# Narrow expert program first and with the rest of the kernel inside its branch; attention scores as 64x64 tiles from the keys as loaded

## The chip, the cores and the metric

The kernel runs on one core of a Trainium2 chip. A core has five engines with instruction queues of their own: TensorE (PE, matrix products; its weight loads are shown as PEld), VectorE (DVE), ScalarE (ACT), GpSimd (POOL) and SyncE (SP, which here only issues DMAs). They meet by semaphores alone. On-chip data lies in SBUF (128 partitions); matrix products go to PSUM (8 banks of 512 fp32 per partition). The metric is the device time of one execution in microseconds.

## What is computed

Three layers in fp32. First a linear attention with a decayed state (B, H, S, D = 2, 8, 768, 48):

```python
for t in range(S):
    cur = np.einsum('bhd,bhe->bhde', u[None] * kt, vt)
    y[:, :, t] = np.einsum('bhd,bhde->bhe', rt, state + cur)
    state = w[None, :, :, None] * state + np.einsum('bhd,bhe->bhde', kt, vt)
```

Its 1536 tokens of 384 features go to a mixture of 8 experts (384 to 1024 and back, relu), each token to the expert of its largest gate logit, at most 384 tokens an expert, times its gate probability:

```python
h = np.maximum(np.einsum('ecd,edf->ecf', disp, w1), 0.0)
y = np.einsum('ecf,efd->ecd', h, w2)
out[i] = gate_w[i] * y[expert_idx[i], pos[i]]
```

Last comes a dense layer over all tokens, 384 to 2048 and back:

```python
h = x @ w_in
r = np.maximum(h, 0.0)
return ((r * r) @ w_out).astype(np.float32)
```

## The kernel before

**Attention** goes over 12 chunks of 128 tokens (6 for each of 2 batches, in turn; four slots of buffers). For a chunk, POOL multiplies the keys in place by a table of decays (L376, k_decayed) and writes the decayed r to Rd (L377, r_decayed), then khat (L383) and ru (L385). Heads lie in pairs: the one on partitions 0 to 47, the other on 64 to 111. ACT copies the decayed keys to Kb, where each head of a pair has a block of its own with zeros in the other's partitions (two copies a chunk, kb_ready; Kb[0] is cleared once by DVE at L773, Kb[1] by POOL at L370). PE then makes vT x wg (L445, three products), the scores (L451, eight fp32 products, 112 partitions deep and 128 x 128 large, into two banks ps_a), the new state (L459) and the outputs (L467, L469). DVE masks the scores to am (L828, one operation for each bank), makes ru, csum and cv (L832, L833, L835), takes the outputs out of PSUM (x_sb L821, heads_l L839) and adds up the states St (L845). PE's L459 waits for St of the chunk before, L467 for am, DVE's L821 for L469. An fp32 product stands in the trace as two weight loads and two matmuls (passes): "x16" is eight products.

**Routing** follows on DVE and PE: positions, the gather indices gidx, the number of tokens of the fullest expert (peaki, L895, count_ready) and each expert's first column (starti, L898).

**The experts** exist as two programs: wide, for experts of up to 384 tokens, and narrow, for up to 240. Every engine but SP reads peaki into a register and branches (by_peak, L280); these inputs take the narrow program. In `moe` POOL gathers each expert's tokens (L393) and, behind the gathers of expert 1, clears the compact arrays yhi and ylo (L412, L413; 128 x 4608 each). The expert outputs are written there column range by column range, 240 or 384 wide, in the order of experts, so that a later expert overwrites what the one before wrote past its own tokens. PE starts with matmuls that only keep it busy (warm: L543, 18 and 6), and transposes the first gathered rows (L592). ACT copies them to xshi, DVE makes the difference xslo (L993). DVE's part starts with gates() (L902 to L906) and the first weight split (L812: wlo = raw - whi), and then come xslo 0 to 2, splits 1 and 2 and the first hlo (L952). For each of 32 units (a quarter of an expert) PE does a hidden product of 18 matmuls (L504) and an output product of 18 (L517), the hidden product one unit ahead. SP loads the weights of a unit (raw, 768 KB) into a ring of four as soon as DVE has split the ones that lay there (w_lo).

**The dense layer** has 24 units over yhi and ylo (L504, L527). Last, POOL scatters the 12 output tiles (L421) and waits for them. This part and the placing matmuls (L616) stand behind the branch, where both programs meet.

The branch reads:

```python
            with eng.If(biggest > NARROW):
                moe(Experts(CAP))
            with eng.Else():
                moe(Experts(NARROW))
```

Of the kernel before, what the change touches and what calls it, by code (L numbers as in the profile page):

```python
# [20 lines left out]
P = 128  # L21
# [36 lines left out]
SLOTS = 4  # L58
NARROW = 240
# [3 lines left out]
def build(nc, feat_d, vT_d, rk_d, vx_d, w_d, u_d, wg_d, wts_d, xd, out):  # L63
    with ExitStack() as ctx:
# [48 lines left out]
        with ExitStack() as a:  # L113
# [5 lines left out]
            Kb = [sb(f"Kb{u}", [P, G, 2, C], F32, a) for u in range(2)]  # L119
# [29 lines left out]
        bank = [ctx.enter_context(nc.psum_tensor(f"bank{j}", [P, 512], F32)) for j in range(8)]  # L149
        ps_a0, ps_a1, ps_y, ps_kv, ps_x, _, ps_tab, ps_tab2 = bank  # L150
        ps_pos = ps_kv
        ps_a = [ps_a0, ps_a1]
# [29 lines left out]
        kb_cleared = sem("kb_cleared")  # L182
        kb_ready = sem("kb_ready")
# [96 lines left out]
        def by_peak(eng, moe):  # L280
# [61 lines left out]
        def _(pool):  # L342
# [27 lines left out]
            nc.gpsimd.memset(Kb[1][:, :, :, :], 0.0).then_inc(kb_cleared, 1)  # L370
# [44 lines left out]
            by_peak(pool, moe)  # L415

            pool.wait_ge(place_ready, 2)
            pool.wait_ge(out_zeroed, 16 * NT)
            for t in range(NT):
                pool.wait_ge(o_dve if t % 2 else o_act, t // 4 * 2 + t % 4 // 2 + 2)  # L420
                nc.gpsimd.indirect_dma_start(  # L421
                    out=out[:, :], out_offset=bass.IndirectOffsetOnAxis(ap=oidx[:, t:t + 1], axis=0),
                    in_=osb[:, t, :], in_offset=None, bounds_check=N - 1, oob_is_err=False).then_inc(scattered, 16)
            pool.wait_ge(scattered, 16 * NT)
# [3 lines left out]
        def _(pe):  # L428
# [9 lines left out]
            with pe.Fori(0, NC_ // 2) as i:  # L438
                for u in range(SLOTS):
                    n, b = 4 * i + u, u % 2  # L440

                    pe.wait_ge(in_vT[u], 16 * (i + 1))
# [20 lines left out]
                    for g in range(G):  # L463
# [4 lines left out]
                        for o in range(2):  # L468
                            mm = pe.matmul(pair, am[:, g // 2, (2 * (g % 2) + o) * C:(2 * (g % 2) + o + 1) * C],  # L469
# [141 lines left out]

            pe.wait_ge(count_ready, 1)
            by_peak(pe, moe)
            for t in range(NT):
                pe.wait_ge(onehot, NT + t + 1)
                mm = pe.matmul(ps_tab2[:, 0:PARTS * NT], onehb[:, t, :], tokv[:, t, :, :].rearrange("p a t -> p (a t)"),  # L616
                               start=(t == 0), stop=(t == NT - 1))
            mm.then_inc(tab_psum, 1)

            def mlp_chunk(t, last):  # L620
                for v in range(MQ):
                    n = MOE_UNITS + MQ * t + v
                    if not (last and v == MQ - 1):
                        pe.wait_ge(w_lo, n + 2)
                        hidden((v + 1) % RING, ps_h[(v + 1) % 2], *compact(t + (v + 1) // MQ), CHUNK)
                    pe.wait_ge(h_ready, 2 * n + 2)
                    if v == 0:
# [470 lines left out]
```

## Time and profile before

| | us |
|---|---|
| median of 3 runs | 461.97 |
| lowest and highest | 461.69, 467.37 |
| profiled execution | 461.56 |
| span of its instructions | 459.8 |
| PE busy in the span | 424.0 (92%) |
| DVE busy | 295.8 (64%) |
| ACT busy | 212.1 (46%) |
| POOL busy | 103.0 (22%) |

The profiled execution takes 461.56 us in all, of which 459.8 us lie between its first and last instruction. All times in the rows are counted from the start of that span. A timeline row reads: start, duration, engine, line, operation, written tile <- read tiles, shape, xcount; in square brackets, how long the engine had been idle and what ended that ("issue": nothing that the profile shows). A matmul's duration holds its way through the array; the distance of two starts is what each costs.

### The profile page before, as it was taken

The numbers are of one execution on the slowest core, as the hardware profiler recorded it, in microseconds if no ns is written. First come the engines' busy times: TensorE is split into PE (matmuls) and PEld (weight loads), VectorE is DVE, ScalarE is ACT, GpSimd is POOL, SyncE is SP. The second block draws the span as 40 slices with busy tenths as digits, with TensorE's granted clock in tenths as the row PEclk, the third lists the DMA queues.
The fourth block names the chain that finished last, engine by engine and source line by source line (L and its number), as shares of the span: only waits on it lengthen the run. The fifth ranks groups of instructions, "written<-read, shape, count | busy, mean of one in ns | idle before, by whom it ended". The sixth has DMA issues, their size and how long they took to land.

```text
span 459.8 us, 8053 instructions
## 1 busy us (share of the span) xinstructions
PE 424.0 (92%) x2922; PEld 399.4 (87%) x2922; DVE 295.8 (64%) x486; ACT 212.1 (46%) x371; POOL 103.0 (22%) x102
## 2 busy tenths in 40 slices
PE   2999999644999999999999999999999999999993
PEld 2999989623999999999999889889899899898993
DVE  8799988759678766676865755455554554554431
ACT  2554665301465555655653644444543445444321
POOL 6998865057101101100000000000300001100003
PEclk9999999957899999999999999999999999999998
DMA  7999982012996456455546323122432142300001
GB/s 201 273 321 296 344 262 112 35 55 65 309 364 227 160 217 233 173 200 199 202 165 209 113 71 136 68 97 110 137 118 88 68 133 93 117 0 1 1 1 69
DMA packets 20477, 69.48 MB, mean 151 GB/s; under 512 B 2840, under 2 KB 9257, under 8 KB 20448
## 3 DMA queue, kind: packets, MB, share of 16 engines
q1 hardware_dynamic: 18656, 64.40, 42.2%
q0 software_dynamic: 1792, 4.72, 2.7%
q8 instruction: 15, 0.25, 0.2%
q14 instruction: 14, 0.11, 0.1%
HBM read 62.82 MB, written 7.08 MB: 152 GB/s over the span
## 4 chain that ended last, share of the span: by engine, by line
PE 79%; DVE 14%; issue 4%; DVEq 1%; POOL 0%; ACT 0%; DMA 0%; ACTq 0%; POOLq 0%
PE bank L504 34%; PE bank L527 22%; PE bank L517 13%; PE bank L469 3%; DVE ru L832 2%; PE bank L451 2%; DVE r_sum L904 2%; PE bank L467 1%; DVE am L828 1%; PE bank L459 1%; DVE cv L835 1%; DVE St L845 1%; PE bank L494 1%; DVE wlo L812 1%; PE bank L445 1%
## 5 line engine op out<-in xcount | busy, mean ns | idle before, releaser
L812 DVE TENSOR_TENSOR wlo<-raw,whi 128x1536 fp32r<-128x1536 f32 x56 | 98.3, 1757 | 91.8 <-ACT whi L642 87.5
L642 ACT ACTIVATE whi<-raw 128x1536 fp32r<-128x1536 f32 x56 | 83.3, 1489 | 83.2 <-PE bank L527 47.6
L421 POOL DMA_INDIRECT out<-osb,oidx x12 | 13.0, 1080 | 247.8 <-ACT osb L755 245.4
L527 PE MATMUL bank<-whi,hhi 128*128 128x384 f32 x192 | 65.0, 338 | 0.5 <-DVE hlo L962 0.5
L527 PE MATMUL bank<-whi,hlo 128*128 128x384 f32 x192 | 64.9, 338 | 0.0
L527 PE MATMUL bank<-wlo,hhi 128*128 128x384 f32 x192 | 64.8, 338 | 0.0
L504 PE MATMUL bank<-xshi,whi 128*128 128x240 f32 x192 | 53.9, 281 | 6.5 <-DVE xslo L993 6.5
L504 PE MATMUL bank<-yhi,whi 128*128 (+1 forms) x144 | 56.9, 395 | 0.0
L504 PE MATMUL bank<-yhi,wlo 128*128 (+1 forms) x144 | 56.9, 395 | 0.0
L504 PE MATMUL bank<-ylo,whi 128*128 (+1 forms) x144 | 56.8, 395 | 0.0
L504 PE MATMUL bank<-xslo,whi 128*128 128x240 f32 x192 | 53.8, 280 | 0.0
L504 PE MATMUL bank<-xshi,wlo 128*128 128x240 f32 x192 | 53.8, 280 | 0.0
L699 ACT ACTIVATE rl<-bank 128x512 f32<-128x512 f32 x48 | 28.6, 600 | 54.5 <-PE bank L504 51.0
L958 DVE TENSOR_TENSOR sq<-rl 128x512 f32<-128x512 f32 x48 | 32.9, 689 | 30.0 <-ACT rl L699 30.0
L504 PEld LDWEIGHTS bank<-xshi,whi 128*128 128x128 f32 x192 | 37.4, 195 | 6.8 <-DVE wlo L812 6.8
L393 POOL DMA_INDIRECT xg<-attention_out,gidx x16 | 18.3, 1142 | 93.1 <-PE bank L494 69.0
L527 PEld LDWEIGHTS bank<-whi,hhi 128*128 128x128 f32 x192 | 36.0, 188 | 1.9 <-issue 0.9
L504 PEld LDWEIGHTS bank<-xshi,wlo 128*128 128x128 f32 x192 | 37.3, 194 | 0.0
L504 PEld LDWEIGHTS bank<-xslo,whi 128*128 128x128 f32 x192 | 37.3, 194 | 0.0
L527 PEld LDWEIGHTS bank<-wlo,hhi 128*128 128x128 f32 x192 | 36.0, 188 | 0.9
L527 PEld LDWEIGHTS bank<-whi,hlo 128*128 128x128 f32 x192 | 36.0, 188 | 0.0
L517 PE MATMUL bank<-hhi,whi 128*128 128x240 f32 x192 | 33.0, 280 | 0.0
(158 smaller groups left out, 794.6 us busy)
## 6 DMA issues: line engine op xcount, KB each, us to landing
raw<-in_wts SPq DMA_DIRECT2D x56, 768.0 KB, 4.2
feat<-in_feat SPq DMA_DIRECT2D x12, 448.0 KB, 6.4
rk<-in_rk SPq DMA_DIRECT2D x12, 384.0 KB, 5.9
vx<-in_vx SPq DMA_DIRECT2D x12, 224.0 KB, 6.5
vT<-in_vT SPq DMA_DIRECT2D x12, 192.0 KB, 6.0
attention_out<-x_sb SPq DMA_DIRECT2D x12, 192.0 KB, 2.8
out<-rl SPq DMA_DIRECT2D x12, 192.0 KB
xg<-attention_out,gidx POOLq DMA_INDIRECT x16, 4.7
```

The lines of the kernel that those rows point to most:

```text
L393: nc.gpsimd.indirect_dma_start(out=xg[e % 2][:, q, :], out_offset=None, in_=xd[:, :], in_offset=bass.IndirectOffsetOnAxis(ap=gidx[:, e * C ...
L421: nc.gpsimd.indirect_dma_start(out=out[:, :], out_offset=bass.IndirectOffsetOnAxis(ap=oidx[:, t:t + 1], axis=0), in_=osb[:, t, :], in_offs ...
L451: mm = pe.matmul(ps_a[g // 2][:, (2 * (g % 2) + o) * C:(2 * (g % 2) + o + 1) * C], Kb[u % 2][0:ROWS, g, o, :], Rd[u][0:ROWS, g * C:(g + 1) ...
L469: mm = pe.matmul(pair, am[:, g // 2, (2 * (g % 2) + o) * C:(2 * (g % 2) + o + 1) * C], vb[u % 2][:, g, o, :], start=False, stop=(o == 1))
L504: mm = pe.matmul(banks[ft][:, 0:width], w[:, r, cols], x(k), start=(k == 0 and step == 0), stop=(k == KT - 1 and step == 2))
L517: mm = pe.matmul(ps_e[dt][:, 0:width], w[:, r, cols], x[:, par, ft, 0:width], start=(q == 0 and ft == 0 and step == 0), stop=(q == EQ - 1 ...
L527: mm = pe.matmul(ps_o[tt][:, 0:DM], x[:, par, ft, tt * P:(tt + 1) * P], w[:, r, cols], start=(v == 0 and ft == 0 and step == 0), stop=(v = ...
L642: return nc.scalar.activation(dst, src, ACT.Copy)
L699: nc.scalar.activation(rl[:, ft, :], banks[ft][:, :], ACT.Relu).then_inc(h_relu, 1)
L812: v.tensor_tensor(wlo[:, r, :], raw[:, r, :], whi[:, r, :].bitcast(F32), ALU.subtract).then_inc(w_lo, 1)
L832: after(v.tensor_tensor(ru[u][:, :], ru[u][:, :], rk[u][:, 1, :], ALU.mult))
L958: v.tensor_tensor(sq[:, ft, :], rl[:, ft, :], rl[:, ft, :], ALU.mult).then_inc(h_sq, 1)
```

## The change

1. In by_peak the narrow program stands first, directly behind the compare, and the wide one behind it. All that follows the experts (placing, dense layer, scatter) moves into a function `rest(x)` on each engine, called inside both branches, so it exists twice.
2. POOL clears yhi and ylo only in the wide program, and only there does ACT wait for it (y_cleared).
3. Kb, its two clears and its ACT copies are gone. PE takes the scores from the keys as decayed in place (feat): for each pair of heads and each head the product is split in two of 64 key columns. A product uses 48 partitions (from 0 or from 64) and writes 64 PSUM partitions (0 to 63 or 64 to 127); the two heads write to different banks. Scores so take 16 products and four banks. The mask reads two banks in one operation. PE waits for k_decayed and r_decayed ahead of the first product of the chunk.
4. The other attention banks move accordingly (ps_tab to bank 1, ps_y, ps_kv and ps_x to 4, 5 and 6).

```diff
-        ps_a0, ps_a1, ps_y, ps_kv, ps_x, _, ps_tab, ps_tab2 = bank
+        ps_a = [ctx.enter_context(nc.psum_tensor(f"score_banks{j}", [P, 2, 512], F32)) for j in range(2)]
+        bank = [ps_a[j][:, o, :] for j in range(2) for o in range(2)]
+        bank += [ctx.enter_context(nc.psum_tensor(f"bank{j}", [P, 512], F32)) for j in range(4, 8)]
+        _, ps_tab, _, _, ps_y, ps_kv, ps_x, ps_tab2 = bank
...
-            with eng.If(biggest > NARROW):
-                moe(Experts(CAP))
+            with eng.If(biggest < NARROW + 1):
+                rest(Experts(NARROW))
             with eng.Else():
-                moe(Experts(NARROW))
+                rest(Experts(CAP))
...
-            nc.gpsimd.memset(Kb[1][:, :, :, :], 0.0).then_inc(kb_cleared, 1)
...
-                    if e == 1:
+                    if e == 1 and x.tiles > 2:
                         nc.gpsimd.memset(yhi[:, :, 0:N].bitcast(F32), 0.0).then_inc(y_cleared, 1)
                         nc.gpsimd.memset(ylo[:, :, 0:N].bitcast(F32), 0.0).then_inc(y_cleared, 1)
...
+                    pe.wait_ge(k_decayed, n + 1)
+                    pe.wait_ge(r_decayed, n + 1)
                     pe.wait_ge(in_vT[u], 16 * (i + 1))
...
-                    pe.wait_ge(kb_ready, 2 * n + 2)
-                    pe.wait_ge(r_decayed, n + 1)
                     for g in range(G):
-                        for o in range(2):
-                            mm = pe.matmul(ps_a[g // 2][:, (2 * (g % 2) + o) * C:(2 * (g % 2) + o + 1) * C],
-                                           Kb[u % 2][0:ROWS, g, o, :], Rd[u][0:ROWS, g * C:(g + 1) * C], start=True, stop=True)
+                        for half in (slice(0, HALF), slice(HALF, P)):
+                            for o in range(2):
+                                rows = slice(ODD * o, ODD * o + D)
+                                mm = pe.matmul(ps_a[g // 2][half, o, (g % 2) * C:(g % 2 + 1) * C],
+                                               feat[u][rows, 1, g * C + half.start:g * C + half.stop],
+                                               Rd[u][rows, g * C:(g + 1) * C], start=True, stop=True)
...
-                for o in range(2):
-                    rows = slice(ODD * o, ODD * o + D)
-                    copy(Kb[u % 2][rows, :, o, :], chunk_view(feat[u][rows, 1, :])).then_inc(kb_ready, 1)
...
-                    act.wait_ge(y_cleared, 2)
+                    if x.tiles > 2:
+                        act.wait_ge(y_cleared, 2)
...
-            v.memset(Kb[0][:, :, :, :], 0.0).then_inc(kb_cleared, 1)
...
-                    v.tensor_tensor(chunk_view(am[:, o, :]), chunk_view(ps[:, :]),
-                                    before[:, :].unsqueeze(1).to_broadcast([P, G, C]), ALU.mult).then_inc(masked, 1)
+                    v.tensor_tensor(am[:, o, :].rearrange("p (o g s) -> p o g s", o=2, g=2),
+                                    ps[:, :, 0:2 * C].rearrange("p o (g s) -> p o g s", g=2),
+                                    before[:, :].unsqueeze(1).unsqueeze(1).to_broadcast([P, 2, 2, C]), ALU.mult).then_inc(masked, 1)
```

PE's program in a chunk of attention, before (bank stands for any PSUM bank):

```order
L445 MATMUL bank<-wg,vT 128x64 x3
L447 ISA
L451 MATMUL bank<-Rd,Kb 128x128 x8
L456 REGISTER_ALU
L459 MATMUL bank<-vx,khat 112x112 x4
```

and in the changed kernel:

```order
L448 MATMUL bank<-wg,vT 128x64 x3
L454 MATMUL score_banks<-Rd,feat 64x128 x16
L460 REGISTER_ALU
L461 ISA
L463 MATMUL bank<-vx,khat 112x112 x4
```

Eight products of full size became sixteen of half the columns. What PE finds behind the branch on the peak count, before (384 is the width of the wide program; the narrow one comes 658 rows further down):

```order
L282 TENSOR_LOAD peaki
L282 ISA x2
L283 COMPARE_AND_BRANCH
L543 MATMUL bank<-match,ones_b 128x288 x18
L592 MATMUL bank<-ident,xg 128x128 x6
L543 MATMUL bank<-match,ones_b 128x288 x6
L603 MATMUL bank<-ident,xg 128x128 x3
L504 MATMUL bank<-xshi,whi 128x384
```

and in the changed kernel, where the narrow program (240) is there at once:

```order
L281 TENSOR_LOAD peaki
L281 ISA x2
L282 COMPARE_AND_BRANCH
L547 MATMUL bank<-match,ones_b 128x288 x18
L596 MATMUL bank<-ident,xg 128x128 x6
L547 MATMUL bank<-match,ones_b 128x288 x6
L508 MATMUL score_banks<-xshi,whi 128x240
```

The same swap stands on DVE, ACT and POOL. POOL's program behind its branch in the changed kernel; the clears of yhi and ylo stand in the wide part, behind the jump to the end:

```order
L282 COMPARE_AND_BRANCH
L391 DMA xg<-attention_out,gidx 128x384 x14
L420 DMA out<-osb,oidx 1536x384 x12
L282 UNCONDITIONAL_BRANCH
L391 DMA xg<-attention_out,gidx 128x384 x4
L410 MEMSET yhi 128x3x1536
L411 MEMSET ylo 128x3x1536
```

The narrow part now ends in the scatters and a jump over the wide part.

## Rows read from the trace of the kernel before

**Rows 1.** Busy time by stage: stretch, length, busy us (count) by engine, clock, DMA.
```profile
9.80:88.00 78.20, 75.46 (x648) 74.39 (x648) 68.38 (x128) 40.28 (x106) 56.69 (x48) 1.00 0.79 245
96.40:112.45 16.05, 5.50 (x30) 3.73 (x31) 11.07 (x8) 0.94 (x3) 14.80 (x9) 0.71 0.18 52
119.40:253.50 134.10, 133.91 (x1181) 132.50 (x1179) 93.11 (x158) 75.65 (x127) 11.35 (x10) 1.00 0.63 218
258.60:452.40 193.80, 193.78 (x972) 175.72 (x972) 97.08 (x118) 84.25 (x118) 10.49 (x10) 1.00 0.23 78
```

**Rows 2.** Timeline of the handoff from routing to the experts, all engines.
```profile
95.70 0.15 DVE L895 CAST peaki<-peak 128x1 int32<-128x1 f32 x1
...
96.27 0.17 DVE L898 CAST starti<-start 128x8 int32<-128x8 f32 x1
...
100.43 3.80 PEld L543 LDWEIGHTS bank<-match,ones_b 128*128 128x128 bf16 x18 [5.60 <-issue]
...
101.29 0.25 DVE L902 TENSOR_REDUCE r_sum<-ex 128x12 f32<-128x96 f32 x1 [4.84 <-issue]
101.58 8.14 DVE L904 TENSOR_SCALAR r_sum<-r_sum 128x12 f32<-128x12 f32 x1
101.85 3.95 POOL L412 MEMSET yhi<- 128x4608 f32 x1
...
104.38 0.82 PE L592 MATMUL bank<-ident,xg 128*128 128x128 f32 x6
...
105.02 0.94 ACT L642 ACTIVATE xshi<-bank 128x256 fp32r<-128x256 f32 x3 [13.32 <-PE bank L592]
...
110.21 1.76 DVE L812 TENSOR_TENSOR wlo<-raw,whi 128x1536 fp32r<-128x1536 f32 x1
...
111.89 1.08 DVE L993 TENSOR_TENSOR xslo<-bank,xshi 128x256 fp32r<-128x256 f32 x3
...
112.45 0.54 PE L504 MATMUL bank<-xshi,whi 128*128 128x240 f32 x1 [6.52 <-DVE xslo L993]
...
119.39 0.58 PE L517 MATMUL bank<-hhi,whi 128*128 128x240 f32 x3
```

**Rows 3.** Timeline of attention: PE in chunks 1, 5, 6, 8, 11; POOL.
```profile
18.42 0.79 PE L445 MATMUL bank<-wg,vT 128*128 128x64 f32 x6
...
43.44 0.79 PE L445 MATMUL bank<-wg,vT 128*128 128x64 f32 x6
...
44.07 2.00 PE L451 MATMUL bank<-Rd,Kb 112*128 112x128 f32 x16
...
45.91 0.95 PE L459 MATMUL bank<-vx,khat 128*112 128x112 f32 x8
...
49.37 0.79 PE L445 MATMUL bank<-wg,vT 128*128 128x64 f32 x6
...
50.82 1.28 POOL L376 TENSOR_TENSOR feat<-feat,Tk 112x512 f32<-112x512 f32 x1 [2.11 <-DMA feat<-in_feat]
...
63.33 2.00 PE L451 MATMUL bank<-Rd,Kb 112*128 112x128 f32 x16
...
81.32 0.79 PE L445 MATMUL bank<-wg,vT 128*128 128x64 f32 x6
```

**Rows 4.** Groups of instructions in attention by line: busy us, mean ns.
```profile
L832 DVE TENSOR_TENSOR ru<-ru,rk 128x384 f32<-128x384 f32 x12 | 14.8, 1234 | 0.0
```

**Rows 5.** The same line's instructions: shortest, median and longest in ns.
```profile
L832 DVE TENSOR_TENSOR ru<-ru,rk x12: 548/818/2969, 15.5 to 84.6; 128x384 f32<-128x384 f32 x12
```

**Rows 6.** Timeline at the start of expert 1: DVE behind a register load of starti.
```profile
154.38 1.76 DVE L812 TENSOR_TENSOR wlo<-raw,whi 128x1536 fp32r<-128x1536 f32 x1 [0.99 <-DVE tokv L934]
```

**Rows 7.** A stretch of 0.4 us in the handoff, columns as in rows 1.
```profile
100.80:101.20 0.40, 0.40 (x4) 0.22 (x3) 0.00 (x0) 0.00 (x0) 0.35 (x1) 0.50 0.00 0
```

**Rows 8.** Waits in attention: who for whom, us, times, longest.
```profile
ACT vx L642 <- PE bank L445: 27.0, 12, 4.1
```

**Rows 9.** Timeline of the end: POOL's last scatter.
```profile
454.49 0.98 POOL L421 DMA_INDIRECT out<-osb,oidx  x1 [0.30 <-issue]
```

More of the change, by code:

```diff
@@ L58 @@
 SLOTS = 4
+HALF = P // 2
 NARROW = 240
@@ L610, in moe @@
                 expert_pair(E // 2 - 1, True, x)
-            pe.wait_ge(count_ready, 1)
[L613 to L627, printed above, removed]
-                        pe.wait_ge(place_ready, 2)
-                        pe.wait_ge(y_ready, E + 1)
-                        pe.wait_ge(o_act, 2 * t + 1)
-                        pe.wait_ge(o_dve, 2 * t + 1)
-                    mlp_out(v % RING, v % 2, v)
@@ L634, in _, with rest, mlp_chunk @@
-            with pe.Fori(0, NCH - 1) as t:
-                mlp_chunk(t, False)
-            mlp_chunk(NCH - 1, True)
+            def rest(x):
+                moe(x)
+                for t in range(NT):
+                    pe.wait_ge(onehot, NT + t + 1)
+                    mm = pe.matmul(ps_tab2[:, 0:PARTS * NT], onehb[:, t, :], tokv[:, t, :, :].rearrange("p a t -> p (a t)"),
+                                   start=(t == 0), stop=(t == NT - 1))
+                mm.then_inc(tab_psum, 1)
+                def mlp_chunk(t, last):
+                    for v in range(MQ):
+                        n = MOE_UNITS + MQ * t + v
+                        if not (last and v == MQ - 1):
+                            pe.wait_ge(w_lo, n + 2)
+                            hidden((v + 1) % RING, ps_h[(v + 1) % 2], *compact(t + (v + 1) // MQ), CHUNK)
+                        pe.wait_ge(h_ready, 2 * n + 2)
+                        if v == 0:
+                            pe.wait_ge(place_ready, 2)
+                            pe.wait_ge(y_ready, E + 1)
+                            pe.wait_ge(o_act, 2 * t + 1)
+                            pe.wait_ge(o_dve, 2 * t + 1)
+                        mlp_out(v % RING, v % 2, v)
+                with pe.Fori(0, NCH - 1) as t:
+                    mlp_chunk(t, False)
+                mlp_chunk(NCH - 1, True)
@@ L639, in _ @@
+            pe.wait_ge(count_ready, 1)
+            by_peak(pe, rest)
         @block.scalar
@@ L1010, in _, with rest @@
             counted = steps.n
[L1012 removed]
+            def rest(x):
                 steps.n = counted
                 moe(x)
[L1016 to L1020 removed]
@@ new lines, in rest, with mlp_chunk @@
+                v.tensor_tensor(gout[:, :], ps_tab2[:, 4 * NT:5 * NT], gout[:, :], ALU.add).then_inc(place_ready, 1)
+                square_lo(MOE_UNITS, 0)
+                def mlp_chunk(t, last):
+                    for q in range(MQ):
+                        n = MOE_UNITS + MQ * t + q
+                        if not (last and q >= MQ - 3):
+                            split_lo(n + 3, (q + 3) % RING)
+                        if not (last and q == MQ - 1):
+                            square_lo(n + 1, (q + 1) % 2)
+                    for tt in (1, 3):
+                        if tt == 1:
+                            dve.wait_ge(o_psum, 3 * t + tt + 1)
+                        else:
+                            dve.wait_ge(unit_done, n + 2)
+                        v.tensor_scalar(osb[:, bass.ds(4 * t + tt, 1), :].rearrange("p a n -> p (a n)"), ps_o[tt][:, 0:DM],
+                                        gout[:, bass.ds(4 * t + tt, 1)], None, ALU.mult).then_inc(o_dve, 1)
@@ L1045 @@
+                with dve.Fori(0, NCH - 1) as t:
+                    mlp_chunk(t, False)
+                mlp_chunk(NCH - 1, True)
+            by_peak(dve, rest)
 def kernel(r, k, v, w, u, moe_w_gate, moe_w1, moe_w2, moe_capacity, moe2_w_in, moe2_w_out):
```

102 lines of the change are left out of this document (39 added, 63 removed).

## The prediction

> **What bounds the kernel now.** I read the stages first, then the handoff between routing and the experts, then one attention chunk. TensorE (PE) is busy 75.46 of 78.20 us in attention, 133.91 of 134.10 us in the expert loop and 193.78 of 193.80 us in the final layers, but only 5.50 of 16.05 us in the handoff from 96.40 to 112.45 us [rows 1]. So in the last two stages only fewer matmuls would help, and the change touches none of those. The handoff is mostly a wait.
>
> The handoff, in order [rows 2]. The peak count (peaki) is there at 95.70 + 0.15 = 95.85 us, starti at 96.44 us. PE needs only the count and starts its warming matmuls (L543) at 100.43, so 4.58 us later; VectorE (DVE) starts its next work (L902) at 101.29, 4.85 us later. Nothing else is waited for: both lie between the branch on the count and the first instruction of the taken side. Then DVE's L904, a 12-element operation, lasts 8.14 us and ends at 109.72; GpSimd (POOL) clears yhi from 101.85 on for 3.95 us and ylo as long behind it, to 109.68. DVE gets free as POOL's clears end. Behind L904 stand the first weight split (1.76 us) and the three xslo (1.08 us), and PE, whose transposes were done at 105.20 and whose second warming ended at 105.93, waits 6.52 us for the first xslo and starts the first hidden product at 112.45. The first expert output (L517) starts at 119.39.
>
> Attention. A chunk's row of PE work repeats every 49.37 - 43.44 = 5.93 us where nothing holds it: 0.63 us of L445, 1.84 us of scores (44.07 to 45.91), the rest 3.46 us of L459, L467 and L469 [rows 3]. From chunk 1 to chunk 11 it takes 62.90 us, a mean of 6.29 us: in some chunks DVE holds PE. DVE's ru product takes 1234 ns in the mean [rows 4], but 548 ns at the shortest and 2969 at the longest [rows 5]: it is stretched while POOL's own products run, and so, less, is cv behind it. A DVE chunk, by adding its operations, is about 5.0 us free and 5.87 us with the mean stretch of the two.
>
> **The change, part by part.**
>
> 1. *The clears of yhi and ylo leave the narrow program.* L904 takes 0.17 us like its neighbours rather than 8.14, and DVE is free for the first split about 8.0 us earlier. The work is then no longer last: PE's own chain is. With the branch as before, warming ends at 104.25, transposes at 105.20, ScalarE's (ACT) first xshi 105.02 + 0.31, its xslo 0.36 later, and the second warming ends at 105.93. The first hidden product would start near 105.95, 6.5 us earlier.
>
> 2. *The narrow program follows the branch directly.* Before, the wide program (658 rows on PE, 203 on DVE as the order prints them) stands between branch and narrow program. The trace has no untaken branch of this kind, so I bound it. From below: a register load at an expert's start costs at most 0.99 us of DVE idleness [rows 6]; the branch also needs a load, two small sequencer operations and the compare. From above: 4.58 us, no gain. I take 2.0 us, twice the row that is nearest, and get warming at 97.85 on PE and L902 at 98.4 on DVE, a gain of 2.6 and 2.9 us.
> The Trainium skill (Runtime: NRT & Kernel Launch, "Instruction fetch mechanics") says that prefetch is sequential and that a taken branch out of the window costs a fetch before execution goes on. By it the whole difference between 4.6 us and a short sequencer path would go; this trace agrees in that both engines lose nearly the same time with nothing pending.
>
> 3. *What is late next in the handoff.* Warming from 97.85 ends at 101.65. The two first gathers are in by then: the DMA share is 0.00 from 100.80 to 101.20 [rows 7], after the second was issued at 97.94 and before the next two move. Transposes (0.82 us) and the second warming end at 103.15; xshi, xslo: the first hidden product at about 103.05. DVE then has 1.08 us of xslo, less the first 0.36, and 1.76 us for weight split 1: hidden product 1 starts at 105.55, takes 18 matmuls at 133.91/1181 = 0.113 us [rows 1], 2.04 us, and four transposes (0.5 us) behind it put the first expert output at 108.1 instead of 119.39. That is **11.3 us**; with part 2 at nothing, 8.4. The clock helps: granted is 0.71 in the mean of the handoff [rows 1], so PE ran at 1.2 GHz for part of it, and again after the wait of 6.52 us; the new order has no wait of that length behind the warming. The weights of unit 4 are asked for by SyncE after split 0, now about 100.5, limited by the gathers at 101.2; hidden product 4 comes near 117.6, so 16 us cover a transfer of 4.2 us.
>
> 4. *Kb goes.* 24 ACT copies of 0.62 us fall, and one clear each on DVE and POOL. At nothing: ACT waits 27.0 us in 12 chunks for PE in front of vx [rows 8], which hides its copies, and both clears end ahead of the first loads that their engines wait for (wcol, feat). PE now waits for k_decayed and r_decayed ahead of L445; in that wait L445 and all behind it are queued. POOL decays chunk 8's keys from 50.82 on and PE takes its scores at 63.33 [rows 3], so the wait costs nothing; if that lead of some 10 us went, each microsecond would go to PE directly. The first chunk is no exception: its L445 starts behind tokw, which is later than both.
>
> 5. *Scores as 16 products of 48x64 by 48x128, in place of 8 of 112x128.* Each fp32 product is two passes in the trace (192 for 96), at 1.84/16 = 0.115 us a pass. No row shows a partly used array running two products at once, so I bound. Below: four tiles fully side by side, 8 x 0.115 = 0.92 us. Above: none side by side, 32 x 0.115 = 3.68 us. In between: passes start in order and the two of a product share a tile, so that only the second pass of one overlaps the first of the next: 17 x 0.115 = 1.95 us. I take 1.95 (nearest to the row's 1.84, as the strict order of passes is what the trace shows), which makes the PE chunk 6.04 rather than 5.93 us. Where DVE holds PE the difference is absorbed; it counts in the six or seven chunks where PE holds itself: 6.5 x 0.11 = **+0.7 us**. At each change between whole and partly used array the overlap of neighbouring passes may be lost too: sixteen passes last 2.00 us at 0.115 us distance, so one lasts 0.275, an exposed one costs 0.16, and 24 of them 3.8 us. I leave that to the range.
> The Trainium skill (TensorEngine Tiling (Array Packing), "Tiling Modes" and "Theoretical Speedup") says that four 64x64 tiles are independent, but that a change of mode drains the engine. By the first, scores would take 0.92 us; by the second, each chunk would pay twice, which speaks against the change. The trace has no such switch; no run here shows either yet.
>
> 6. *PSUM banks move, the mask reads two banks in one pattern.* 512 elements in either case: nothing. *The tail is inside the branch.* At the join nothing is idle before, so nothing is won. At the end POOL jumps over the wide program behind its last wait, which comes after the last scatter [rows 9], and nothing covers that: between nothing and the 3 us or so that the first branch may lose to its jump; I take **+0.3**, since POOL's wide part is short (22 gathers, 2 clears, 12 scatters).
>
> Sum: 461.6 (the profiled execution, 459.8 span and 1.8 around it) - 11.3 + 0.7 + 0.3 = 451.3; the median of the runs is 0.4 above the profiled one, so **451.7 us**.
>
> **Rivals.**
> - *Full overlap of the tiles.* Scores 0.92 us and 0.32 us for two exposed passes: PE chunk 5.3 us; DVE's 5.87 us bounds. Stage: 11 x (6.29 - 5.87) = 4.6 us less. 451.7 - 0.7 - 4.6 = 446.4 us. For it: the four products use rows and columns of their own. Against: the passes come in pairs on one tile.
> - *No overlap (the other side).* Scores 3.68 us: 12 x 1.84 = 22.1 us more, 62.90 - 59.3 = 3.6 of it absorbed where DVE held PE, 16 more passes at the first chunk's half clock (+1.8), exposed passes up to 3.8. 451.0 + 20.3 to 24.1 = 471.3 to 475.1 us, slower. It takes the whole gain from scores of about 3.0 us a chunk on. For it: the trace has never two products at once, and nothing forces them.
> - *The branch costs what it cost.* Then 8.4 us and not 11.3: 454.6 us, within 2%.
> - *The stretch moves.* With other phases POOL may hold DVE's ru and cv more (2.97 us was the longest ru): +3 us, 454.7.
>
> **How the numbers follow.** Forecast 0.40, full overlap 0.25, no overlap 0.12, branch unchanged 0.12, stretch or end jump 0.11. Faster by over 2% means under 452.7; 2% is about what this kernel's measurement can tell from no change. Forecast: three quarters of it lies under 452.7 (0.30), full overlap all (0.25), the rest little (0.09): 0.64. Within 2%: 0.24. Slower: 0.12. The range leaves out no overlap and a little of the rest: 445.5 to 457.5.
>
> **What would show it.** L904's successor near 0.17 us, no yhi clear on POOL; the distance from peaki to warming about 2 us (4.6 would refute part 2); the first expert output about 11 us closer to peaki; L454 about 1.95 us a chunk (0.9 to 1.4: full overlap; over 3: none), L448 being L445's new number, its mean distance between 6.2 and 6.5 us; from the last scatter's issue to the end of the span 5.3 us as now, or up to 3 more for the jump. The forecast is wrong above all if scores cost over 3.0 us a chunk.

## The result and the profile after

The kernel before takes 462.11 us (median of 4 runs, 461.69 to 467.37), the changed one 449.37 us (median of 4 runs, 444.03 to 455.65). A fifth execution on record took 449.95 us. The ratio is 0.964, with a 95% interval from 0.952 to 0.976: faster. Ratios, here and below, compare only the executions on record as fast, and for the changed kernel that leaves out 453.22 and 455.65 us, so that a ratio need not be that of the medians (here 0.972). Forecast were 451.7 us and a range from 445.5 to 457.5. The median lies in the range, but the ratio, times 462.11, is 445.3 us, just below its end; the executions spread over 11.6 us, and why they do was in no step of the forecast. The profiled execution of the changed kernel, 455.65 us with a span of 453.9, is the slowest of them.

A further series of the same changed kernel, taken with the later experiments (label after_again), gave 451.96 us (4 runs, 451.12 to 455.37) beside 462.79 us of before (7 runs), ratio 0.980, interval 0.974 to 0.985: a gain of about 2%, which this series alone doesn't put clearly above 2%.

> The changed kernel once more, for a second trace. Theory (its time is spread by how often VectorE's ru or cv is held by POOL's products for about 3 us in attention, after which TensorE runs a chunk at a granted clock of 0.5): between 444 us with no such chunk and 456 us with two; each chunk with a distance of about 10.5 us instead of 5.65 accounts for 4.8 us. Rival (the spread comes from another stage, such as the weights' transfers): the distances of L448 are the same as in the first trace and the difference lies behind the peak count.

The rival is refuted: as the table shows, the two profiled executions differ in attention (90.4 and 85.1 us), not behind the peak count. The theory's one price doesn't hold: no distance is near 10.5 us in this trace, but two are long, 7.90 and 9.35 us from L448 to L448.

Here is where the time went, from the spans of three traces. Attention is counted from PE's first product of chunk 0 to the end of peaki, the handoff from there to the first expert output.

| us | before | after, profiled | after_again, profiled |
|---|---|---|---|
| start to PE's first product of chunk 0 | 9.8 | 9.4 | 10.9 |
| attention and routing | 86.0 | 90.4 | 85.1 |
| handoff to the first expert output | 23.5 | 12.0 | 11.6 |
| experts, dense layer, to the last matmul's end | 333.0 | 333.2 | 333.4 |
| last matmul's end to the end of the span | 7.4 | 8.9 | 8.4 |
| span | 459.8 | 453.9 | 449.4 |

**Stages.** The same four stretches as [rows 1], read from the profiled execution of the changed kernel: stretch, length, busy us (count) of PE, PEld, DVE, ACT, POOL, granted clock, DMA share, GB/s.

```profile
9.36:91.00 81.64, 75.85 (x839) 70.52 (x839) 66.19 (x125) 26.73 (x82) 55.47 (x48) 0.92 0.75 235
100.00:111.00 11.00, 10.07 (x62) 8.00 (x63) 7.41 (x13) 2.01 (x6) 9.24 (x7) 0.73 0.46 136
118.00:253.00 135.00, 134.00 (x1158) 131.44 (x1158) 95.39 (x166) 78.46 (x133) 10.43 (x10) 1.00 0.63 212
258.00:446.00 188.00, 187.02 (x939) 169.66 (x937) 93.31 (x114) 80.66 (x113) 11.13 (x11) 1.00 0.23 77
```

PE is now busy in 10.07 of 11.00 us of the handoff, where it was 5.50 of 16.05 [rows 1]. Experts and dense layer are as full as they were. What is new is in the first row: the clock granted in attention is 0.92 and was 1.00.

**The handoff.** Timeline of all engines, columns as in [rows 2].

```profile
99.66 0.15 DVE L901 CAST peaki<-peak 128x1 int32<-128x1 f32 x1
...
100.86 4.50 PE L547 MATMUL bank<-match,ones_b 128*128 128x288 bf16 x18 [1.94 <-issue]
101.51 0.25 DVE L908 TENSOR_REDUCE r_sum<-ex 128x12 f32<-128x96 f32 x1 [1.10 <-issue]
101.80 0.17 DVE L910 TENSOR_SCALAR r_sum<-r_sum 128x12 f32<-128x12 f32 x1
...
102.91 0.43 POOL L398 MEMSET rl<- 128x384 f32 x1
103.43 1.76 DVE L817 TENSOR_TENSOR wlo<-raw,whi 128x1536 fp32r<-128x1536 f32 x1 [0.99 <-POOL rl L398]
103.50 2.56 POOL L391 DMA_INDIRECT xg<-attention_out,gidx  x1 [0.17 <-issue]
...
107.12 0.35 PE L508 MATMUL score_banks<-xshi,whi 128*128 128x240 f32 x1
...
111.83 0.58 PE L521 MATMUL bank<-hhi,whi 128*128 128x240 f32 x3
```

Peaki is there at 99.81. PE starts warming 1.05 us later (before 4.58), DVE goes on 1.10 us after starti (before 4.85), and L910, the old L904, takes 0.17 us (before 8.14) [rows 2]. The first expert output follows peaki by 12.02 us instead of 23.54.

**A chunk.** Timeline of PE. The last row, with x4, is from a window that ends 0.05 us after the scores' first start.

```profile
40.18 0.79 PE L448 MATMUL bank<-wg,vT 128*128 128x64 f32 x6
40.90 1.10 PE L454 MATMUL score_banks<-Rd,feat 48*64 48x128 f32 x32
42.04 1.04 PE L463 MATMUL bank<-vx,khat 128*112 128x112 f32 x8
...
45.83 0.79 PE L448 MATMUL bank<-wg,vT 128*128 128x64 f32 x6
```

```profile
40.90 0.34 PE L454 MATMUL score_banks<-Rd,feat 48*64 48x128 f32 x4
```

All 32 passes are through in 1.10 us; from their first start to that of L463 are 1.14 us, where the scores of before took 1.84 [rows 3]. Four passes have started within the first 0.05 us. The chunk's distance is 45.83 - 40.18 = 5.65 us and was 5.93.

**Two chunks at half clock.** Of chunk 2, DVE and POOL, then PE, then the granted clock around it (columns as in the stage rows).

```profile
22.22 1.59 POOL L374 TENSOR_TENSOR feat<-feat,Tk 112x512 f32<-112x512 f32 x1
23.29 3.18 DVE L841 TENSOR_TENSOR cv<-vx,csum 128x448 f32<-128x448 f32 x1
23.76 1.27 POOL L375 TENSOR_TENSOR Rd<-feat,T 112x512 f32<-112x512 f32 x1
24.99 1.00 POOL L381 TENSOR_TENSOR khat<-rk,tokw 128x384 f32<-128x384 f32 x1
25.96 1.37 POOL L383 TENSOR_TENSOR ru<-rk,ub 128x384 f32<-128x384 f32 x1
```

```profile
24.00 0.79 PE L448 MATMUL bank<-wg,vT 128*128 128x64 f32 x6
...
28.09 1.83 PE L463 MATMUL bank<-vx,khat 128*112 128x112 f32 x8 [2.27 <-DVE St L851]
...
34.52 0.79 PE L448 MATMUL bank<-wg,vT 128*128 128x64 f32 x6
```

```profile
24.00:27.30 3.30, 1.82 (x40) 1.51 (x38) 3.23 (x4) 0.89 (x3) 3.30 (x4) 1.00 0.77 237
27.30:34.00 6.70, 5.91 (x29) 5.91 (x29) 4.08 (x8) 1.23 (x4) 6.70 (x7) 0.50 0.90 271
```

DVE's cv, 0.72 us in the next chunk, lasts 3.18 us here. POOL's products run back to back, and cv ends at 26.47, 0.48 us after khat's end at 25.99: it sat out the rest of one POOL product and two whole ones. The fourth, L383, starts at 25.96 and takes 1.37 us where it takes 1.00 otherwise, so that here POOL gives way to cv. The new state St is late by that, and PE idles 2.27 us in front of L463. The granted clock is then 0.50, which is 1.2 instead of 2.4 GHz, up to 34.0, and L463 takes 1.83 us instead of 1.04. The chunk takes 34.52 - 24.00 = 10.52 us in place of 5.65. Chunk 7 does it again, there with ru held (3.02 us), PE idle for 2.12 us ahead of L463 at 62.26 and 68.67 - 58.31 = 10.36 us from L448 to L448. Both together cost 9.6 us.

### The profile page after: what moved, and what is told of

Same layout as the page of the kernel before. It is cut to its first block, busy times and chain, and to the rows that moved or that the text cites. A ratio compares the mean times of both kernels' runs of the same rounds, so it can differ in the third digit from the quotient of the medians.

```text
span 453.9 us, 8402 instructions
## 1 busy us (share of the span) xinstructions
PE 423.1 (93%) x3114; PEld 394.0 (87%) x3114; DVE 284.4 (63%) x485; ACT 198.0 (44%) x347; POOL 95.5 (21%) x99
## 4 chain that ended last, share of the span: by engine, by line
PE 84%; DVE 9%; issue 3%; POOL 1%; DMA 0%; DVEq 0%; ACT 0%; POOLq 0%; ACTq 0%
PE score_banks L508 34%; PE bank L531 22%; PE bank L521 13%; PE bank L473 4%; PE bank L463 3%; PE bank L471 3%; PE score_banks L454 2%; DVE cv L841 1%; DVE ru L838 1%; PE bank L547 1%; PE bank L448 1%; PE bank L498 1%; DVE am L833 1%; DVE St L851 1%; DVE ylo L987 0%
## 5 line engine op out<-in xcount | busy, mean ns | idle before, releaser
L508 PE MATMUL score_banks<-yhi,whi 128*128 (+1 forms) x144 | 56.9, 395 | 0.0
L508 PE MATMUL score_banks<-ylo,whi 128*128 (+1 forms) x144 | 56.8, 394 | 0.0
L508 PE MATMUL score_banks<-yhi,wlo 128*128 (+1 forms) x144 | 56.8, 394 | 0.0
L508 PE MATMUL score_banks<-xshi,whi 128*128 128x240 f32 x192 | 52.8, 275 | 0.1
L508 PE MATMUL score_banks<-xslo,whi 128*128 128x240 f32 x192 | 52.7, 274 | 0.0
L508 PE MATMUL score_banks<-xshi,wlo 128*128 128x240 f32 x192 | 52.7, 274 | 0.0
L508 PEld LDWEIGHTS score_banks<-xshi,whi 128*128 128x128 f32 x192 | 36.2, 188 | 0.5 <-issue 0.3
L508 PEld LDWEIGHTS score_banks<-xshi,wlo 128*128 128x128 f32 x192 | 36.2, 189 | 0.0
L508 PEld LDWEIGHTS score_banks<-xslo,whi 128*128 128x128 f32 x192 | 36.2, 188 | 0.0
L473 PE MATMUL bank<-vb,am 128*128 128x112 f32 x192 | 33.1, 300 | 0.0
```

The lines of the kernel that those rows point to most:

```text
L473: mm = pe.matmul(pair, am[:, g // 2, (2 * o + g % 2) * C:(2 * o + g % 2 + 1) * C], vb[u % 2][:, g, o, :], start=False, stop=(o == 1))
L508: mm = pe.matmul(banks[ft][:, 0:width], w[:, r, cols], x(k), start=(k == 0 and step == 0), stop=(k == KT - 1 and step == 2))
```

## The experiments

All medians of one table stand beside those of the kernel before on the same chip.

| run | us (median, runs) | before | ratio, 95% interval |
|---|---|---|---|
| only_clears | 454.46 (4) | 461.64 | 0.984, 0.979 to 0.990 |
| only_branch | 452.63 (4) | 461.64 | 0.980, 0.974 to 0.986 |
| no_tiles | 452.82 (4) | 461.64 | 0.982, 0.976 to 0.987 |
| only_tiles | 462.24 (12) | 461.64 | 0.993, 0.989 to 0.998 |
| free_products | 445.34 (4) | 462.79 | 0.962, 0.958 to 0.966 |
| same_tile | 452.62 (1) | 462.79 | none, one execution |
| best | 442.72 (4) | 462.79 | 0.957, 0.954 to 0.961 |
| before_free | 458.65 (10) | 461.51 | 0.996, 0.992 to 1.001 |
| rows_only | 442.03 (4) | 461.51 | 0.966, 0.960 to 0.972 |

**Which edit gives the handoff?** Only the clears' edit, on the kernel before (ACT's wait for the clears goes with it):

```diff
-                    if e == 1:
+                    if e == 1 and x.tiles > 2:
```

> The kernel before with one edit: yhi and ylo are cleared in the wide program alone. Theory (the clears held VectorE, and PE's own chain is next): L904 falls from 8.14 us to about 0.2, the first hidden product starts near 105.95 us instead of 112.45, the first expert output comes 8.4 us earlier, total 461.7 - 8.4 = 453.3 us. Rival (VectorE was held by something else, such as code that was not there): L904 stays long, no change, 461.7 us.

Timeline of the handoff in only_clears:

```profile
96.12 0.15 DVE L896 CAST peaki<-peak 128x1 int32<-128x1 f32 x1
...
100.68 4.50 PE L543 MATMUL bank<-match,ones_b 128*128 128x288 bf16 x18 [5.31 <-issue]
...
111.77 0.59 PE L517 MATMUL bank<-hhi,whi 128*128 128x240 f32 x3
```

With the clears gone and the branch as it was, warming still starts 100.68 - 96.27 = 4.41 us behind peaki, but the first expert output follows peaki by 15.50 us and not 23.54: 8.0 us. The forecast's sum had 8.4. The next run has the branch's order and the tail inside it, but clears and Kb as before. Against the changed kernel, without the lines that bring Kb back:

```diff
-                    if e == 1 and x.tiles > 2:
+                    if e == 1:
...
-                    if x.tiles > 2:
-                        act.wait_ge(y_cleared, 2)
+                    act.wait_ge(y_cleared, 2)
```

> The changed kernel with the clears of yhi and ylo back and the scores taken from Kb in whole products as before; what is left of the change is the order of the two programs and the tail inside the branch. Theory: PE and VectorE start 3.5 us earlier behind the branch (1.05 us from the peak count to the first warming matmul, as in the changed kernel's trace), but POOL's clears start at the same time and end at the same time, so the first hidden product does not come earlier, and the jump at the end costs 1.5 us: 461.7 + 1.5 = 463.2 us. Rival (the branch counts by itself): 461.7 - 3.5 + 1.5 = 459.7 us.

Both expectations were wrong. Timeline of the handoff in only_branch:

```profile
95.62 0.15 DVE L905 CAST peaki<-peak 128x1 int32<-128x1 f32 x1
...
96.85 4.50 PE L547 MATMUL bank<-match,ones_b 128*128 128x288 bf16 x18 [1.97 <-issue]
97.48 0.25 DVE L912 TENSOR_REDUCE r_sum<-ex 128x12 f32<-128x96 f32 x1 [1.11 <-issue]
97.76 0.17 DVE L914 TENSOR_SCALAR r_sum<-r_sum 128x12 f32<-128x12 f32 x1
...
103.33 3.97 POOL L413 MEMSET yhi<- 128x4608 f32 x1
103.65 3.42 DVE L822 TENSOR_TENSOR wlo<-raw,whi 128x1536 fp32r<-128x1536 f32 x2
...
107.94 0.58 PE L521 MATMUL bank<-hhi,whi 128*128 128x240 f32 x3
```

The branch alone brings the first expert output from 23.54 to 12.17 us behind peaki, nearly the 12.02 of both edits together. DVE passes its small in-place operation (L914) at 97.76, 5.6 us before POOL's first clear starts, and what it does beside the clears is not held by them: two weight splits take 3.42 us at 103.65, 1.71 each, as alone. So not DVE's work but one DVE operation was held, a tensor_scalar from SBUF to SBUF, and either edit gets it out of the clears' way. The edits' gains, 8.0 and 11.4 us, don't add up.

The Trainium skill (SBUF — State Buffer, "Who interferes with whom") says that GpSimd and a VectorE operation in a two-port mode lock each other out for a whole instruction, and that a VectorE operation with two SBUF inputs is locked out only by a GpSimd one that reads SBUF. A clear reads nothing, and the traces agree: the splits take 1.71 us beside a clear, L904 took 8.14. That L904 ran in such a mode no row shows.

The next kernel differs from only_branch by the clears alone (and ACT's wait for them):

```diff
-                    if e == 1:
+                    if e == 1 and x.tiles > 2:
```

> The changed kernel with the scores taken from Kb in whole products as before: both edits of the handoff, none of attention. Theory: the handoff from the peak count to the first expert output takes 12.0 us as in the changed kernel instead of 23.5, the jump at the end costs 1.5: 461.7 - 11.5 + 1.5 = 451.7 us. Rival (the gain of the changed kernel lies in attention alone): above 456 us.

No_tiles takes 452.82 us, only_branch 452.63: with the branch in order, taking the clears out is worth nothing that can be measured. Their first expert output follows peaki by 12.2 us in both.

**What are the tiles worth alone?** The kernel before with the new attention and nothing else of the change:

```diff
+                    pe.wait_ge(k_decayed, n + 1)
+                    pe.wait_ge(r_decayed, n + 1)
...
-                    pe.wait_ge(kb_ready, 2 * n + 2)
...
+                        for half in (slice(0, HALF), slice(HALF, P)):
```

> The kernel before with the new attention alone: scores in 64x64 tiles from the keys as decayed, no Kb. Theory (the 32 passes run about four at a time, 1.1 us a chunk instead of 1.84, and VectorE's chain is then the bound at about 5.65 us a chunk): where TensorE keeps its full clock, 461.7 - 7.5 = 454.2 us; each chunk in which a VectorE product is held for 3 us costs about 4.8 us more, since PE idles over 2 us and its granted clock falls to 0.5 for the chunk; with two such chunks 463.9 us. Rival (passes of one product exclude each other, scores near 1.95 us a chunk): 462.4 us with no spread.

The 12 executions lie between 455.21 and 469.30 us, with a median of 462.24: as fast as before in the middle, and 7 us to either side. The trace has one chunk at half clock, in which PE idled for 2.66 us:

```profile
29.04 1.83 PE L460 MATMUL bank<-vx,khat 128*112 128x112 f32 x8 [2.66 <-DVE St L841]
```

Its free chunks take 5.65 us, its scores 1.10. So the tiles save time in each free chunk, and in many executions waits seem to take it back; only one of the 12 left a trace. The theory came near both ends (454.2 us with nothing held, 463.9 with two held chunks). Its rival gave the median, 462.4 us, but for a wrong reason: it had scores of 1.95 us and no spread. In the profiled execution of only_clears, which has the old scores, one chunk was held and slowed too (cv 3.18 us, PE idle 2.04 us, 9.74 us for the chunk), while the longest idle time of PE in attention in the trace of before is 1.05 us. That makes the hold older than the tiles. With them it cost more: for the same cv of 3.18 us the chunk was 3.8 us over its free length in only_clears (9.74 - 5.94) and 4.9 in the changed kernel (10.52 - 5.65). That the tiles are the reason is not shown by one pair.

**Is it POOL that holds DVE?** The changed kernel, with one operand of ru and cv taken out of SBUF, so that neither reads both from there:

```diff
+        ps_key = ps_tab2[:, 0:DM]
+        csum = ps_tab2[:, DM:DM + H]
...
+                act.wait_ge(x_ready, n + 1)
+                copy(ps_key, rk[u][:, 1, :]).then_inc(key_copied, 1)
...
-                after(v.tensor_tensor(ru[u][:, :], ru[u][:, :], rk[u][:, 1, :], ALU.mult))
+                dve.wait_ge(key_copied, n + 1)
+                after(v.tensor_tensor(ru[u][:, :], ru[u][:, :], ps_key, ALU.mult))
```

> The changed kernel, with VectorE's two products of two SBUF operands in attention freed of that: ScalarE copies k into PSUM for the product with ru, and csum lies in PSUM. Theory (POOL's products hold only a VectorE product that reads both operands from SBUF, and the holds cause the idle time and the lower clock): ru takes 0.55 us and cv 0.65 us in every chunk, every distance of L448 behind the first is near 5.65 us, the granted clock in attention is 1.00, the time is 444 us or a little less with little spread. Rival (holds come from memory traffic of the loads, whatever the operands): ru still reaches 2 us and more, and the spread stays.

Groups of DVE in attention (busy us, mean ns), first of the changed kernel as in after_again, then of free_products, and a last row with PE's busy time and the clock over 60 us of free_products:

```profile
L838 DVE TENSOR_TENSOR ru<-ru,rk 128x384 f32<-128x384 f32 x12 | 12.9, 1073 | 0.0
L841 DVE TENSOR_TENSOR cv<-vx,csum 128x448 f32<-128x448 f32 x12 | 11.1, 928 | 0.4
```

```profile
L846 DVE TENSOR_TENSOR cv<-vx,bank 128x448 f32<-128x448 f32 x12 | 7.4, 620 | 0.4
L843 DVE TENSOR_TENSOR ru<-ru,bank 128x384 f32<-128x384 f32 x12 | 6.5, 544 | 0.0
```

```profile
20.00:80.00 60.00, 59.79 (x754) 54.55 (x754) 50.08 (x109) 27.00 (x86) 44.23 (x41) 1.00 0.85 276
```

Ru falls from 1073 to 544 ns and cv from 928 to 620 in the mean, PE is busy for 59.79 of 60.00 us, every chunk after the first takes 5.63 to 5.66 us and the clock stays at 1.00. The kernel takes 445.34 us, 6.6 less than after_again on the same chip, and its executions lie within 1.7 us (444.12 to 445.81). No single ru or cv takes over 0.63 us. The theory holds. The same edit on the kernel before:

> The kernel before with one edit in attention alone: ACT copies each chunk's keys into PSUM bank 7, DVE's ru product reads them there, and csum lies in the same bank, so that neither ru nor cv has both of its operands in SBUF. Theory (POOL's own products hold such a DVE operation, and a held one makes PE wait): ru falls from a mean of 1234 ns to about 550 and cv from 814 to about 620, and the longest ru from 2969 ns to about 700, every chunk after the first takes 5.93 to 5.95 us instead of a mean of 6.29, so 11 x 0.35 = 3.8 us less: about 458 us, ratio near 0.992. Rival (the stretch comes from the data that the loads write into SBUF, or from DVE's own queue): ru and cv keep their means within 10%, and the time stays at 461 to 462 us.

```profile
L840 DVE TENSOR_TENSOR cv<-vx,bank 128x448 f32<-128x448 f32 x12 | 7.4, 621 | 0.4
L837 DVE TENSOR_TENSOR ru<-ru,bank 128x384 f32<-128x384 f32 x12 | 6.5, 544 | 0.0
```

These are the two groups in before_free; every chunk after the first takes 5.94 us. The hold worked both ways: from 15 to 80 us POOL's own ru takes 1004 ns in the mean and took 1124 before, its Rd 1277 and 1408. The time is 458.65 us beside 461.51, 2.9 less, though the interval of the ratio (0.992 to 1.001) holds no change as well. In the traces, the ten distances from chunk 1 to chunk 11 add up to 62.9 us before and 59.4 in before_free, to 67.2 in the profiled changed kernel, 63.3 in after_again and 56.4 in free_products. So the holds cost 3.5 us in the old kernel's trace, and 10.8 and 6.8 us in the two of the tiled one. Free of holds, the tiles bring 5.94 - 5.64 = 0.30 us a chunk.

**How do the passes run side by side?** Two orders were tried. First, on the changed kernel, the loops turned so that the same quarter of the array is used twice in a row:

```diff
-                    for g in range(G):
+                    for two in range(G // 2):
                         for half in (slice(0, HALF), slice(HALF, P)):
                             for o in range(2):
+                                for g in (2 * two, 2 * two + 1):
```

> The changed kernel with the order of its sixteen score products altered: the two products that use the same quarter of the array follow each other. Theory (passes start in program order, and one that finds its quarter busy holds all behind it): the groups of four passes break up, scores cost 0.11 us times about 24 steps, 2.6 us a chunk, and the distance of L448 grows to about 7.1 us. Rival (each quarter has its own queue): 1.1 us a chunk as before, distance 5.65 us.

```profile
35.28 1.17 PE L455 MATMUL score_banks<-Rd,feat 48*64 48x128 f32 x32
```

In this timeline of PE the scores take 1.17 us and not 1.10, and chunks that nothing holds take 5.64 us. The theory is refuted, and the rival fits: each quarter of the array works on its own passes, and the order in which they are issued hardly counts. On which quarter a pass runs no row shows. The kernel's 452.62 us come from two chunks of 8.65 and 10.91 us, whose PE idled 1.58 and 2.47 us for St.

Second, on the best kernel (below), the scores split by rows alone, 8 products of 48 x 128:

```diff
-                        for half in (slice(0, HALF), slice(HALF, P)):
-                            for o in range(2):
...
+                        for o in range(2):
```

> Like the kernel called best, but the scores are split by rows alone: 8 products 48 deep and 128 columns wide (16 passes) in place of 16 products of 64 columns, heads on partitions 0 to 47 and 64 to 111 in turn, into different banks. Theory (products on rows of their own run side by side whatever their columns, so here two at a time): passes start in pairs about 0.109 us apart, 8 pairs make again 0.87 us from first to last start and about 1.1 us of PE a chunk, and the chunk keeps its distance of 5.4 us: about 442.7 us. Rival (only passes with rows and columns of their own overlap, 128 columns wide ones run one behind the other): 16 x 0.109 = 1.75 us from first to last, 0.87 us more a chunk, distance 6.3 us, about 452 us.

PE in a chunk of rows_only; the last row is from a window that ends 0.06 us after the scores' first start:

```profile
40.16 0.79 PE L447 MATMUL bank<-wg,vT 128*128 128x64 f32 x6
40.89 1.16 PE L452 MATMUL score_banks<-Rd,feat 48*128 48x128 f32 x16
...
45.56 0.79 PE L447 MATMUL bank<-wg,vT 128*128 128x64 f32 x6
```

```profile
40.89 0.38 PE L452 MATMUL score_banks<-Rd,feat 48*128 48x128 f32 x2
```

Sixteen passes take 1.16 us, two at a time, and the chunk again 5.40 us. Two halves of rows do for this shape what four quarters do, with half the instructions. The time, 442.03 us, is that of best: on their two chips they take 0.958 and 0.957 of the medians of before.

**A version that is faster than both.** Free_products with two more edits. DVE's sum of the gate logits, which stood between the new state and the next mask, goes behind the next chunk's masks. And POOL alone keeps its scatters behind the branch:

```diff
+                if n:
+                    store_logits(n - 1)
                 dve.wait_ge(ru_ready, n + 1)
...
-                store_logits(n)
+            store_logits(NT - 1)
...
-            by_peak(pool, rest)
+            by_peak(pool, moe)
```

> free_products with two more edits: POOL's scatters stand behind both branches again, so that its jump over the wide program lies long before the end, and VectorE adds up the logits of a chunk (0.3 us) after the masks of the next instead of before. Theory: the tail is 1.3 us shorter (last matmul to end 7.5 us instead of 8.8), the distance of L448 falls from 5.65 to about 5.45 us, bound by TensorE: 444 - 1.3 - 2.2 = 440.5 us. Rival (the loop is bound elsewhere, or the end waits for something other than POOL): free_products' time, about 443.5 us.

It takes 442.72 us (440.83 to 442.96), 2.6 less than free_products. A chunk takes 5.41 us and not 5.64: PE's chunk was bounded by the loop over DVE (outputs, state, logits, mask), and 0.27 us of logits were in it; in free_products PE's loads for L473 waited up to 0.2 us for am in each chunk, in best they don't. The end fell short of its expectation, 0.4 us and not 1.3. POOL's last scatter in the changed kernel and in best, and a late stretch of each in which no engine works and only an access of a DMA could be left:

```profile
447.14 0.98 POOL L420 DMA_INDIRECT out<-osb,oidx  x1 [0.30 <-issue]
```

```profile
450.20:453.80 3.60, 0.00 (x0) 0.00 (x0) 0.00 (x0) 0.00 (x0) 0.00 (x0) 0.50 0.01 2
```

```profile
433.04 0.98 POOL L421 DMA_INDIRECT out<-osb,oidx  x1 [0.30 <-issue]
```

```profile
436.04:439.04 3.00, 0.00 (x0) 0.00 (x0) 0.00 (x0) 0.00 (x0) 0.00 (x0) 0.50 0.00 0
```

From the last scatter's start to the end of the span it is 6.8 us in the changed kernel, 6.4 in free_products, 6.1 in best and 5.3 in the kernel before [rows 9]. The six traces of kernels with POOL's scatters inside the branch give 6.1 to 6.8 us (6.5 in the mean), best and rows_only 6.1 and 5.8, the four kernels with everything behind the branch 5.3 to 5.4. The changed kernel moves some 7 KB (3.60 us at 2 GB/s) in a stretch where none of its own transfers is left; its DMA view has one packet of the instruction queue there, best has none. So POOL's jump over the wide program costs about half a microsecond, a difference no larger than the spread of the six. Another half is in best too, where PE, DVE and ACT still jump; what it is was not tried.

## Why the prediction was right or wrong

1. **The clears (part 1)**: right in place and size. L910 takes 0.17 us, and alone the edit gives 8.0 us (sum: 8.4).
2. **The branch (part 2)**: right in kind, the gain too small. Branch and load cost 1.05 us on PE and not 2.0 (before 4.58): the gain is 3.5 us, forecast 2.6. The rival by which the branch costs what it did is refuted.
3. **What is late next (part 3)**: the sum held, 11.5 us measured, 11.3 forecast, out of errors that cancel. Warming comes 0.95 us earlier than assumed, but lasts 4.50 us, all of it at a granted clock of 0.50, where the forecast took 3.8 from the row of its weight loads (PE's own was 4.11), and the first split waits 0.99 us for POOL's clear of rl. That the sum came out so well was partly luck. What the forecast never asked is whether the order of the branch alone would end the hold: it did, as only_branch showed, because one operation was held and not all of DVE's work. With the thought that DVE is free only when the clears end, that run should have been slower than before.
4. **Kb and the new waits (part 4)**: right in size, wrong for the first chunk. There PE does wait for the decays in the profiled execution:

```profile
9.36 1.52 PE L448 MATMUL bank<-wg,vT 128*128 128x64 f32 x6 [1.65 <-POOL Rd L375]
```

   It cost nothing, since the product still starts 0.47 us earlier than before (9.83), and in after_again it waits for tokw, as forecast. No later chunk waits for them.
5. **The scores (part 5)**: this is the step that failed. "Passes start in order and the two of a product share a tile, so that only the second pass of one overlaps the first of the next" gave 1.95 us; measured are 1.14 from the scores' start to the next product's, and four passes have started within the first 0.05 us. The rival of full overlap had the scores right, 0.92 us and 0.32 for the changes of shape, 1.24 in all; its bound of 5.87 us for the chunk was too high, 5.64 are measured. The change of shape shows in front of the scores: L448 to L454 is 0.72 us where L445 to L451 was 0.63 [rows 3]. The +0.7 us of the sum should have been -6.5: the ten distances from chunk 1 to chunk 11 add up to 62.90 us in the trace of before and to 56.43 in free_products. Of these 6.5 us, 2.9 are the tiles' (before_free has 59.36), and 3.5 are what holds cost before, which the tiles alone don't win back. With the holds gone, 461.6 - 11.5 - 6.5 + 1.5 for the end is 445.1, near which two executions of the changed kernel lie (444.03 and 445.52). That these two had no holds is worked out from this sum, since neither left a trace.
6. **The stretch moves (a rival, 3 us)**: right in place, too small by half. A hold was priced as the stretch of one operation. It is that, and in most cases the clock falls behind it and the rest of the chunk runs at 1.2 GHz: 4.9 and 4.7 us over a free chunk in the profiled execution, 3.7 in after_again, and 2.3 where the clock stayed. All long distances together cost 10.8 us in the first trace (455.65 us, 10.3 above free_products) and 6.8 in the second (451.12), which is as large as the spread. That no step of the forecast followed an idle PE to its clock in attention, although the handoff's part did, is the second failure, and why its one number could not stand for all executions.
7. **The end**: +1.5 us in place of +0.3 in the profiled execution, 0.8 to 1.4 in five other traces with the tail inside the branch. Taken near the lower end of its bounds, it lay nearer the middle.

What stays open: why a hold is there in one execution and not in the next of the same program, and why some idle times bring the clock down and others do not. In after_again PE idled 2.27 us ahead of the L463 at 33.98, and the clock stayed at 1.00; in the same trace it idled 2.10 us ahead of the one at 59.05, and the clock fell, to 0.57 in the mean from 60 to 64 us:

```profile
33.98 1.04 PE L463 MATMUL bank<-vx,khat 128*112 128x112 f32 x8 [2.27 <-DVE St L851]
```

```profile
31.70:36.00 4.30, 2.02 (x18) 1.86 (x17) 4.13 (x9) 1.23 (x4) 4.30 (x5) 1.00 0.82 278
...
60.00:64.00 4.00, 4.00 (x21) 3.92 (x21) 2.26 (x5) 0.26 (x1) 0.91 (x2) 0.57 0.94 284
```

Nor does the length of the idle time decide elsewhere: the clock fell behind 1.58 us in same_tile and stayed at 1.00 behind 1.64 us in no_tiles.

## What to carry to other kernels

When a faster step leaves an engine idle in front of a stretched operation, look at the granted clock behind the idle time: the wait may cost twice its length (2.27 us idle, 4.9 us lost). Move one operand of the stretched VectorE product to PSUM before anything else is tuned around it; here that took the spread away as well as the time. And before adding up the gains of two edits to one wait, ask whether either of them alone ends it.

## What the runs showed of the hardware

- Fp32 passes on rows of their own run side by side, four at a time on 64x64 quarters (32 passes in 1.10 us; 1.17 us with the same quarter twice in a row), two at a time on halves of rows with all 128 columns (16 in 1.16 us). Going to and from partly used rows costs little: from the scores' first start to L463's it is 1.14 us for eight groups, of which 0.9 would be eight of the 0.11 us that a pass costs elsewhere, plus 0.09 us in front of them. The Trainium skill (TensorEngine Tiling (Array Packing), "Key Properties") says that a change of mode drains the engine; the trace allows for some 0.3 us a chunk for both changes.
- A DVE product with both operands in SBUF lasted up to 3.18 us, longer than any one of POOL's products beside it (1.0 to 1.6 us): POOL's next one goes ahead of it. With one operand in PSUM none took over 0.63 us.
- An indirect gather of POOL lasted 2.56 and 2.49 us where it started just behind the start of one of DVE's weight splits, and mostly 1.00 to 1.3 us otherwise. It isn't so each time: in no_tiles one that started 0.03 us behind a split took 1.00.
- A branch not taken, with the load of its register and the compare, cost 1.05 us on PE and 1.10 on DVE; with the jump over the wide program it was 4.58 and 4.85 [rows 2].
